# Token blocks folded out of the accumulation bank, early starts for three sequence groups, and magnitudes of half the second weight summed on ScalarE

## The chip, the cores and the metric

The kernel runs on one core of one Trainium2 chip. The metric is the device time of one execution in microseconds (us). The engines are TensorE (PE in the profile, its weight loads PEld), VectorE (DVE), ScalarE (ACT), GpSimd (POOL) and SyncE (SP, which here only issues DMAs).

## The reference, cut to what matters

Three stages run one after the other on batch 2, sequence 768, 8 heads of 64 features (512 features in all). First a decayed linear attention in blocks, then a mixing stage with a Fourier transform over tokens and features and a two-layer network, then a second two-layer network.

```
for b in range(nb):                                     # attention, blocks with a carried state
    intra = (q_b @ k_b^T) * Dmask ; intra = intra @ v_b
    inter = (q_b * lam_pow) @ kv_state
    out_b = intra + inter
    kv_state = lam_block * kv_state + (k_b * rev_pow)^T @ v_b

X = np.fft.fft(x, axis=1) ; X = np.fft.fft(X, axis=2)   # mixing over tokens, then features
u = x + np.real(X)
un = (u - mean(u)) / sqrt(var(u) + 1e-6)
x = u + np.maximum(un @ w1, 0) @ w2                     # first network, w1 512x2048, w2 2048x512

xn = (x - mean(x)) / sqrt(var(x) + 1e-6) * g
out = x + np.maximum(xn @ w3, 0) @ w4                   # second network
```

## The kernel before, in words

Each engine has its own program, written out by hand in the order in which it runs; engines meet through counting semaphores (`wait_ge`). Nothing reorders the work, so an instruction that waits holds back all that stands behind it on its engine.

**Attention.** The tokens go in 6 blocks of 128 (`c`) for 2 batches (`b`), 12 units `u = 2c + b`. For a unit, TensorE makes the scores (L377), VectorE masks them (`masks`, L921), TensorE updates the state (L390) and computes the output rows (L407, L412) into a bank `xps[b]`, counted by `pv_done`. ScalarE copies the bank to `xlow` (blocks 0 to 2) or `xhigh` (blocks 3 to 5) in `x_rows` (L684, counted by `x_done`) and sends the rows to a DRAM copy `x_dram` (L687); then `expand` (L697) writes the new state. Output rows of unit u may be written only when `x_rows` of unit u-2 has freed the bank.

**Fold.** The Fourier transform over tokens uses the symmetry of the sine and cosine: block `c` of the upper half is added to and subtracted from block `c-3` of the lower half by VectorE (`fold_tokens`, L953 and L954, counted by `sf_done`), and then its features are folded by GpSimd (`fold_features`, L1350 and L1351, counted by `fold_done[b]`) or, for the last block of batch 0, by VectorE (L982 and L983, `fold_last`). VectorE's program runs, for each u: `decay_state(u-1)`, `masks(u)`, `grow_state(u-1)`, `fold_tokens(u-1)`, and `largest(0, u-4)` (L965), the largest magnitude in one of the 8 chunks of the first weight.

**Sequence and feature transforms.** `sequence` runs 16 groups f (8 for each batch), each of 3 matmuls of 385 or 384 columns (L475; one for each of three token blocks), into `f1_bank[f % 3]`. ScalarE copies each group out (`y_columns`, L750 to L752, `y_done`). `features(j)` (L494) and `middle_row` (L516) transform over features; ScalarE copies one half (`q_rows`, L765), VectorE combines (`combine`, L1071 to L1077, `fix_row` L1088), GpSimd adds the other rows (`add_rows`, L1437, `addA`) onto rows that it gathered from `x_dram` (L1422). SyncE loads further rows from `x_dram` (L331 on), after a wait for all of `x_out`.

**Normalising.** VectorE's `statistics` (L1106) for the first 512 tokens waits for `addA` of two tiles, `deviation` (L758) is ScalarE's square root, `normalise` is L1138. TensorE transposes the result in `turn(0, k)` (L544), ScalarE copies it out (`turned`, L775) and makes its half-precision part (`x_hi`, L792); VectorE makes the rest (`x_lo`, L1147) and two sums (`x_sum`).

**Weights.** Weights are scaled by a power of two taken from their largest magnitude. `largest` over 8 chunks, `largest_of_all` (L989), then TensorE turns the column of maxima into a row (`spread_rows`, L523), VectorE takes its maximum (`tops`, L995), TensorE spreads it back (`spread_back`, L528), VectorE copies it (`walls`, L1003) and makes the scale (`power_of_two`, L1010 to L1021, `wsc_ready`). Then `up_hi` (ScalarE, L722 and L723) and `up_lo` (VectorE, L1031 and L1032) split a chunk of the first weight in two halves, from sums that GpSimd makes (`up_sums`, L1380 to L1385); `down_hi` (L739) and `down_lo` (L1039) do so for the second weight.

**The networks.** From `pair(0)` on TensorE runs 32 pairs: 7 products each by a seven-multiplication scheme (L555) and, one pair behind, the second layer (`down`, L575). The chunks of the first weight from 3 on are made inside pairs 1 to 6.

## Time and profile before

| what | value |
|---|---|
| median of 3 runs | 613.15 us (612.04 to 613.87) |
| profiled execution, its own time | 613.28 us |
| its span | 611.5 us |
| PE busy | 593.2 us, 97% of the span |
| DVE busy | 369.4 us, 60% |
| ACT busy | 242.5 us, 40% |
| POOL busy | 146.7 us, 24% |
| mean granted TensorE clock | 0.994 |

The page of the profile names, for each engine, how long it was busy in the span, and in 40 slices of the span how busy it was and which share of full clock TensorE was granted. The answers of the trace go finer: the timeline lists instructions in order of time, merged where they repeat, with the idle time before them and what ended it; the table of stretches gives busy time and granted clock of chosen stretches. A line number is that of the kernel before.

### The profile page before, as it was taken

What the parts mean: (1) busy time and instruction counts of PE and PEld (TensorE: products, weight loads), DVE (VectorE), ACT (ScalarE), POOL (GpSimd) and SP (SyncE); (2) the same over time, 40 slices, a digit from 0 to 9 for tenths busy, and PEclk for the clock granted to TensorE, in tenths of its full rate; (3) what the DMA queues carried; (4) which work ended last, traced back from release to release, by engine and by line L of the source; (5) the groups of instructions that cost most, each with busy time, mean ns of one, the idle gap of its engine ahead of it and who ended that gap; (6) DMA issues with size and microseconds to landing.
All of it is one profiled execution on the core that took longest, in us unless ns stands there. A gap on an engine that the chain in (4) does not pass through costs nothing.

```text
span 611.5 us, 10866 instructions
## 1 busy us (share of the span) xinstructions
PE 593.2 (97%) x4143; PEld 404.3 (66%) x4143; DVE 369.4 (60%) x641; ACT 242.5 (40%) x488; POOL 146.7 (24%) x129
## 2 busy tenths in 40 slices
PE   9998899999999999999989999999999999999997
PEld 4898655776565667666656665666666766666664
DVE  2589779987766765665867897624454333433223
ACT  0232153744555223442456664344332344223221
POOL 1646685154231000103034751002000020000000
PEclk9999799999999999999999999999999999999999
DMA  7999880000000643213022422000010000010001
GB/s 234 395 385 388 292 264 0 2 1 1 2 1 1 178 127 111 86 53 105 18 86 70 135 74 70 0 3 0 1 66 5 1 2 1 22 47 1 1 2 69
DMA packets 41412, 50.43 MB, mean 82 GB/s; under 512 B 2442, under 2 KB 28690, under 8 KB 39956
## 3 DMA queue, kind: packets, MB, share of 16 engines
q1 hardware_dynamic: 39156, 45.05, 22.2%
q10 hardware_dynamic: 1728, 3.15, 1.3%
q0 software_dynamic: 480, 1.57, 0.8%
q8 instruction: 32, 0.52, 0.3%
q14 instruction: 16, 0.13, 0.1%
HBM read 43.46 MB, written 6.30 MB: 81 GB/s over the span
## 4 chain that ended last, share of the span: by engine, by line
PE 71%; DVE 10%; POOL 7%; DMA 5%; ACT 3%; issue 3%; SPq 1%; DVEq 0%; POOLq 0%; ACTq 0%
PE bank L575 33%; PE bank L555 30%; DMA arena<-attn 3%; PE bank L412 2%; DVE arena L1031 2%; PE bank L544 2%; DMA arena<-w 1%; PE bank L407 1%; POOL arena L1381 1%; POOL arena L1380 1%; DVE arena L1172 1%; POOL arena L1422 1%; POOL arena L1383 1%; DVE arena L1032 1%; DVE arena L1039 1%
## 5 line engine op out<-in xcount | busy, mean ns | idle before, releaser
L575 PE MATMUL bank<-arena 128*128 128x512 f16 x1152 | 287.1, 379 | 2.8 <-DVE arena L1180 1.5
L555 PE MATMUL bank<-arena 128*128 128x256 f16 x2016 | 259.4, 273 | 2.4 <-DVE arena L1032 1.8
L555 PEld LDWEIGHTS bank<-arena 128*128 128x128 f16 x2016 | 196.6, 98 | 76.7 <-DVE arena L1032 3.3
L575 PEld LDWEIGHTS bank<-arena 128*128 128x128 f16 x1152 | 112.1, 98 | 89.5 <-DVE arena L1180 1.8
L1172 DVE SCALAR_TENSOR_TENSOR arena<-arena 128x512 f16<-128x512 f32 x96 | 72.2, 752 | 67.6 <-ACT arena L808 67.6
L808 ACT ACTIVATE arena<-arena 128x512 f16<-128x512 f32 x96 | 60.4, 629 | 98.5 <-DVE arena L1213 93.1
L1207 DVE SCALAR_TENSOR_TENSOR arena<-bank,arena 128x256 f32<-128x256 f32 x48 | 20.3, 423 | 77.8 <-PE bank L555 77.8
L854 ACT ACTIVATE arena<-bank 128x256 f32<-128x256 f32 x48 | 18.4, 384 | 63.9 <-PE bank L555 63.9
L1393 POOL TENSOR_TENSOR arena<-arena 128x512 f32<-128x512 f32 x5 | 6.8, 1368 | 146.9 <-ACT arena L779 90.8
L1213 DVE SCALAR_TENSOR_TENSOR arena<-bank,arena 128x256 f32<-128x256 f32 x48 | 20.2, 422 | 30.6 <-PE bank L555 30.6
L965 DVE TENSOR_REDUCE arena<-arena 128x1 f32<-128x1024 f32 x32 | 38.4, 1208 | 0.0
L1147 DVE TENSOR_TENSOR arena<-arena 128x512 f16<-128x512 f32 x42 | 30.1, 728 | 10.4 <-ACT arena L792 10.4
L825 ACT ACTIVATE arena<-bank 128x256 f32<-128x256 f32 x48 | 18.4, 384 | 42.1 <-PE bank L555 42.1
L475 PE MATMUL bank<-arena 128*128 128x385 f32 (+1 forms) x96 | 34.5, 512 | 0.0
L1380 POOL TENSOR_TENSOR arena<-arena 128x256 f32<-128x256 f32 x16 | 14.8, 926 | 66.9 <-DMA arena<-w 64.5
L837 ACT ACTIVATE arena<-bank 128x256 f32<-128x256 f32 x48 | 18.4, 382 | 31.3 <-PE bank L555 31.3
L1196 DVE SCALAR_TENSOR_TENSOR arena<-bank,arena 128x256 f32<-128x256 f32 x48 | 20.1, 418 | 17.4 <-PE bank L555 17.3
L820 ACT ACTIVATE arena<-bank 128x256 f32<-128x256 f32 x48 | 18.2, 379 | 28.0 <-PE bank L555 28.0
L412 PE MATMUL bank<-arena 128*128 128x64 f32 x192 | 27.3, 272 | 0.2 <-DVE arena L921 0.2
L475 PEld LDWEIGHTS bank<-arena 128*128 128x128 f32 x96 | 18.6, 200 | 12.4 <-issue 2.2
L412 PEld LDWEIGHTS bank<-arena 128*128 128x128 f32 x192 | 25.9, 199 | 0.7 <-issue 0.7
L792 ACT ACTIVATE arena<-arena 128x512 f16<-128x512 f32 x42 | 25.7, 624 | 0.0
(101 smaller groups left out, 553.4 us busy)
## 6 DMA issues: line engine op xcount, KB each, us to landing
arena<-w SPq DMA_DIRECT2D x48, 256.0 KB, 4.4
arena<-w SPq DMA_DIRECT2D x24, 512.0 KB, 3.7
arena<-attn SPq DMA_DIRECT2D x10, 1024.0 KB, 8.7
x_dram<-arena ACTq DMA_DIRECT2D x12, 256.0 KB, 6.9
out<-arena SPq DMA_DIRECT2D x12, 256.0 KB, 2.1
arena<-attn SPq DMA_DIRECT2D x4, 512.0 KB, 4.3
arena<-c SPq DMA_DIRECT2D x1, 1153.5 KB, 11.1
arena<-g SPq DMA_DIRECT2D x1, 514.0 KB, 12.7
```

What stands on the lines that cost most here:

```text
L412: last = nc.tensor.matmul(xps[b][:, h * D:(h + 1) * D], PT[b][:, par, pair, :], v, start=first, stop=True, skip_group_check=not first)
L475: last = nc.tensor.matmul(f1_bank[f % 3][:, 0:n], lhs, C1[:, c, par * NE:par * NE + n], start=c == 0, stop=c == HALF - 1)
L555: last = nc.tensor.matmul(bank_, wst[:, i, wx, w, kt, :], xs[s % 2][:, ux, x, kt, :], start=not started and k == 0, stop=k == 5, skip_grou ...
L575: last = nc.tensor.matmul(ops[t][:], hT[n % 2][:, half, hx, t * P:(t + 1) * P], wdn[:, i, wx, half * DM:(half + 1) * DM], start=first and ...
L792: nc.scalar.activation(xs[s % 2][:, 0, which, :, :], x_block(which), ACT.Copy).then_inc(xh_done, 1)
L808: nc.scalar.activation(hT[n % 2][:, half, 0, :], z[n % 2][:, half, :], ACT.Relu).then_inc(hh_done, 1)
L965: nc.vector.tensor_reduce(wmax_chunks[:, m, c:c + 1], raw, AX.X, ALU.max, apply_absolute_value=True).then_inc(wred[m], 1)
L1147: nc.vector.tensor_tensor(xs[s % 2][:, 1, which, :, :], x_block(which), xs[s % 2][:, 0, which, :, :], ALU.subtract).then_inc(xl_done, 1)
L1172: nc.vector.scalar_tensor_tensor(hT[n % 2][:, half, 1, :], z[n % 2][:, half, :], 0.0, hT[n % 2][:, half, 0, :], ALU.max, ALU.subtract).the ...
L1207: nc.vector.scalar_tensor_tensor(z[n % 2][:, 1, 0:HT], seventh[:, 0:HT], H_SCALE, u2, ALU.mult, ALU.add).then_inc(z21_out, 1)
L1213: nc.vector.scalar_tensor_tensor(z[n % 2][:, 1, HT:TOK], a, H_SCALE, p7, ALU.mult, ALU.add).then_inc(z22_out, 1)
L1380: nc.gpsimd.tensor_tensor(s1, a21, a22, ALU.add).then_inc(ws_step, 1)
```

## The change

It does the following.

1. `fold_tokens` reads the upper block straight out of the bank `xps[b]` and waits for `pv_done` rather than `x_done`. `x_rows` of units 6 to 11 in turn waits for `sf_done`, so that the copy frees the bank only after the fold, and `expand` comes ahead of it there.
2. `largest(0, 4..7)` moves from the loop's iterations u = 8 to 11 to behind the loop.
3. The first three sequence groups are written as `first_sequence`: their matmuls over token blocks 0 and 1 come first, those over block 2, which wait for `fold_last`, after them. Matmuls are the same in number and shape.
4. `spread_rows(0, 1)` stands behind group 3 (before: 1), `spread_back(0, 1)` behind group 5 (before: 3). Those of the second weight, `(1, 2)`, move from among groups 9 to 11 to behind group 13 and behind `features(2)`, and to bank 7. `turn(0)` stands behind group 12 (before: 13).
5. `magnitude(4..7)` on ScalarE takes the sums of magnitudes (`Abs` with an accumulated output) of four chunks of the second weight; `largest(1, 4..7)` is gone from VectorE. The sum bounds the largest magnitude from above, so the scale may come out smaller.
6. `up_hi(0, 2)` moves behind `y_columns(11)`, `up_lo(0, 1)` behind `normalise`, `up_lo(0, 2)` to the end of pair 0, `down_hi(0, 0)` into pair 0. `largest_of_all(1)`, `tops(1, 2)`, `walls(1, 2)` and `power_of_two(1)` move to behind `normalise` and among and behind `x_lo`.

```diff
+            def along(f, c):
+                b, par, dk = f // 8, f // 4 % 2, f % 4
+                n = NE if par == 0 else NO
+                lhs = fold[:, b, 2 * par + dk // 2, c, (dk % 2) * P:(dk % 2 + 1) * P]
+                return nc.tensor.matmul(f1_bank[f % 3][:, 0:n], lhs, C1[:, c, par * NE:par * NE + n],
+                                        start=c == 0, stop=c == HALF - 1)
+            def first_sequence():
+                pe.wait_ge(fold_done[0], HALF - 1)
+                for f in range(3):
+                    for c in range(HALF - 1):
+                        along(f, c)
+                for f in range(3):
+                    pe.wait_ge(fold_last, 1 + f // 2)
+                    along(f, HALF - 1).then_inc(f1_done, 1)
             def sequence(groups):
                 for f in groups:
-                    b, par, dk = f // 8, f // 4 % 2, f % 4
-                    if f == 0:
-                        pe.wait_ge(fold_done[b], HALF - 1)
-                        pe.wait_ge(fold_last, 1)
-                    if f == 2:
-                        pe.wait_ge(fold_last, 2)
+                    b = f // 8
                     if f == 8:
                         pe.wait_ge(fold_done[b], HALF)
                     if f >= 3:
                         pe.wait_ge(y_done, f - 2)
-                    n = NE if par == 0 else NO
                     for c in range(HALF):
-                        lhs = fold[:, b, 2 * par + dk // 2, c, (dk % 2) * P:(dk % 2 + 1) * P]
-                        last = nc.tensor.matmul(f1_bank[f % 3][:, 0:n], lhs, C1[:, c, par * NE:par * NE + n],
-                                                start=c == 0, stop=c == HALF - 1)
+                        last = along(f, c)
                     last.then_inc(f1_done, 1)
...
-            sequence(range(2))
+            first_sequence()
+            sequence(range(3, 4))
             pe.wait_ge(id_in, 16)
             pe.wait_ge(ones_done, 1)
             spread_rows(0, 1)
-            sequence(range(2, 4))
+            sequence(range(4, 6))
             spread_back(0, 1)
-            sequence(range(4, F1_FIRST))
...
             features(0)
             middle_row(0)
             features(1)
-            sequence(range(F1_FIRST, F1_FIRST + 1))
+            sequence(range(F1_FIRST, F1_FIRST + 4))
             pe.wait_ge(fix_done, 1)
-            spread_rows(1, 2)
-            sequence(range(F1_FIRST + 1, F1_FIRST + 3))
-            spread_back(1, 2)
-            sequence(range(F1_FIRST + 3, 14))
-            pe.wait_ge(wall_done, 2)
             for k in range(KT):
                 turn(0, k)
-            sequence(range(14, 16))
+            sequence(range(F1_FIRST + 4, F1_FIRST + 5))
             pe.wait_ge(ev_done, NT)
+            spread_rows(1, 2, bank[7])
+            sequence(range(F1_FIRST + 5, 16))
             features(2)
+            spread_back(1, 2, bank[7])
...
                 c, b = divmod(u, B)
                 act.wait_ge(pv_done, u + 1)
+                if c >= HALF:
+                    act.wait_ge(sf_done, u - B * HALF + 1)
                 rows_u = xlow[:, b, c, :] if c < HALF else xhigh[:, c - HALF, b, :]
                 nc.scalar.activation(rows_u, xps[b][:], ACT.Copy).then_inc(x_done, 1)
...
                     act.wait_ge(zeroed, B)
+                act.wait_ge(pv_done, u + 1)
                 act.wait_ge(st_done, u + 1)
...
             for u in range(UNITS):
-                x_rows(u)
-                if u < UNITS - B:
+                if u < B * HALF:
+                    x_rows(u)
                     expand(u)
+                else:
+                    if u < UNITS - B:
+                        expand(u)
+                    x_rows(u)
...
                     if c == 2:
-                        act.wait_ge(fold_done[0], HALF - 1)
-                        act.wait_ge(fold_done[1], HALF)
+                        act.wait_ge(mag_done, SLOTS // 2)
...
+            def magnitude(c):
+                act.wait_ge(w_chunk_in[1][c], 16)
+                if c > SLOTS // 2:
+                    act.wait_ge(mag_done, c - SLOTS // 2)
+                junk = wst[:, 2, 0, 0:4, :, :].rearrange("p b k n -> p (b k n)")
+                nc.scalar.activation(junk, wraw[1][:, c, :], ACT.Abs,
+                                     accum_out=wmax_chunks[:, 1, c:c + 1]).then_inc(mag_done, 1)
...
                 hidden_hi(n, 1)
+                if n == 0:
+                    down_hi(0, 0)
...
             y_columns(7)
+            act.wait_ge(fold_done[0], HALF - 1)
+            act.wait_ge(fold_done[1], HALF)
+            magnitude(4)
             y_columns(8)
+            magnitude(5)
             q_rows(0)
+            magnitude(6)
+            q_rows(1)
+            y_columns(9)
+            magnitude(7)
+            deviation(0)
+            y_columns(10)
+            y_columns(11)
             up_hi(0, 2)
-            q_rows(1)
-            for f in range(9, 12):
-                y_columns(f)
-            deviation(0)
             y_columns(12)
-            y_columns(13)
             for k in range(KT):
                 turned(0, k)
             x_hi(0, 0)
             x_hi(0, 1)
+            x_hi(0, 2)
+            y_columns(13)
+            x_hi(0, 3)
+            x_hi(0, 4)
             y_columns(14)
-            x_hi(0, 2)
-            x_hi(0, 3)
+            x_hi(0, 5)
+            x_hi(0, 6)
             y_columns(15)
-            x_hi(0, 4)
-            x_hi(0, 5)
-            down_hi(0, 0)
-            x_hi(0, 6)
             q_rows(2)
...
             def fold_tokens(u):
                 c, b = divmod(u, B)
-                dve.wait_ge(x_done, u + 1)
+                dve.wait_ge(pv_done, u + 1)
                 if c > HALF + 1:
                     dve.wait_ge(fold_done[b], c - HALF - 1)
                 to = sfold[c % 2]
-                lo, hi = xlow[:, b, c - HALF, :], xhigh[:, c - HALF, b, :]
+                lo, hi = xlow[:, b, c - HALF, :], xps[b][:]
                 nc.vector.tensor_tensor(to[:, b, 0, :], lo, hi, ALU.add)
                 nc.vector.tensor_tensor(to[:, b, 1, :], lo, hi, ALU.subtract).then_inc(sf_done, 1)
...
-                if UNITS - SLOTS <= u < UNITS:
-                    largest(0, u - UNITS + SLOTS)
+                if 2 * B <= u < 2 * B + SLOTS // 2:
+                    largest(0, u - 2 * B)
+            for c in range(SLOTS // 2, SLOTS):
+                largest(0, c)
             def largest_of_all(m):
-                dve.wait_ge(wred[m], SLOTS)
+                if m == 1:
+                    dve.wait_ge(mag_done, SLOTS // 2)
+                dve.wait_ge(wred[m], SLOTS // 2 if m == 1 else SLOTS)
...
                 hidden_lo(n, 0)
+                if n == 0:
+                    up_lo(0, 2)
...
-            for c in range(2, 5):
-                largest(1, c)
+            largest(1, 2)
+            largest(1, 3)
             up_lo(0, 0)
-            largest(1, 5)
-            up_lo(0, 1)
-            largest(1, 6)
-            largest(1, 7)
-            largest_of_all(1)
             combine(0)
             fix_row(0)
             combine(1)
-            tops(1, 2)
             statistics(0, range(NT))
-            walls(1, 2)
             row_scale(0)
             normalise(0, range(NT))
-            up_lo(0, 2)
+            largest_of_all(1)
+            up_lo(0, 1)
             x_sum(0, 0)
             x_sum(0, 1)
             x_lo(0, 0)
             x_lo(0, 1)
             x_sum(0, 2)
-            power_of_two(1)
             x_lo(0, 2)
             x_sum(0, 3)
+            tops(1, 2, bank[7])
             for k in range(3, 7):
                 x_lo(0, k)
+            walls(1, 2, bank[7])
+            power_of_two(1)
             out_scale(0)
```

VectorE's program at the end of the attention loop, before (L921 `masks`, L953 and L954 `fold_tokens`, L965 `largest`, L982 and L983 the last feature fold):

```order
L953 TENSOR_TENSOR arena<-arena 128x512 [waits x_done]
L954 TENSOR_TENSOR arena<-arena 128x512
L965 TENSOR_REDUCE arena<-arena 128x1 [waits w0_in6]
L921 TENSOR_TENSOR arena<-bank,arena 128x512 [waits pv_done,qk_done]
L921 TENSOR_TENSOR arena<-bank,arena 128x512
L953 TENSOR_TENSOR arena<-arena 128x512 [waits fold_done0,x_done]
L954 TENSOR_TENSOR arena<-arena 128x512
L982 TENSOR_TENSOR arena<-arena 128x2x256 [waits sf_done]
L983 TENSOR_TENSOR arena<-arena 128x2x256
L965 TENSOR_REDUCE arena<-arena 128x1 [waits w0_in7]
L953 TENSOR_TENSOR arena<-arena 128x512 [waits fold_done1,x_done]
L954 TENSOR_TENSOR arena<-arena 128x512
```

and with the change (L951 `masks`, L983 and L984 `fold_tokens`, L1012 and L1013 the last feature fold, L995 `largest`; L1023 is `largest_of_all`):

```order
L983 TENSOR_TENSOR arena<-arena,bank 128x512 [waits pv_done]
L984 TENSOR_TENSOR arena<-arena,bank 128x512
L951 TENSOR_TENSOR arena<-bank,arena 128x512 [waits pv_done,qk_done]
L951 TENSOR_TENSOR arena<-bank,arena 128x512
L983 TENSOR_TENSOR arena<-arena,bank 128x512 [waits fold_done0,pv_done]
L984 TENSOR_TENSOR arena<-arena,bank 128x512
L1012 TENSOR_TENSOR arena<-arena 128x2x256 [waits sf_done]
L1013 TENSOR_TENSOR arena<-arena 128x2x256
L983 TENSOR_TENSOR arena<-arena,bank 128x512 [waits fold_done1,pv_done]
L984 TENSOR_TENSOR arena<-arena,bank 128x512
L995 TENSOR_REDUCE arena<-arena 128x1 [waits w0_in4]
L995 TENSOR_REDUCE arena<-arena 128x1 [waits w0_in5]
```

Two more L995 rows and then L1023 follow. The masks of unit 11 follow the fold of unit 9 with no reduction between, the fold reads the bank, and four reductions stand behind the last fold.

TensorE's program from the second `features` to `turn(0)` and on to the last group, before (L475 sequence, L523 `spread_rows`, L528 `spread_back`, L544 `turn`):

```order
L475 MATMUL bank<-arena 128x385 x2
L523 MATMUL bank<-arena 1x128 [waits wmax_done,fix_done]
L475 MATMUL bank<-arena 128x385 [waits y_done]
L475 MATMUL bank<-arena 128x385 x2
L475 MATMUL bank<-arena 128x385 [waits y_done]
L475 MATMUL bank<-arena 128x385 x2
L528 MATMUL bank<-arena 128x1 [waits top_done]
L475 MATMUL bank<-arena 128x384 [waits y_done]
L475 MATMUL bank<-arena 128x384 x2
L475 MATMUL bank<-arena 128x384 [waits y_done]
L475 MATMUL bank<-arena 128x384 x2
L544 MATMUL bank<-arena 128x128 [waits un_done,wall_done]
```

and with the change (L461 sequence, L552 `turn`, L531 `spread_rows`):

```order
L461 MATMUL bank<-arena 128x384 [waits y_done]
L461 MATMUL bank<-arena 128x384 x2
L552 MATMUL bank<-arena 128x128 [waits un_done,fix_done]
L552 MATMUL bank<-arena 128x128 x15
L461 MATMUL bank<-arena 128x384 [waits y_done]
L461 MATMUL bank<-arena 128x384 x2
L531 MATMUL bank<-arena 1x128 [waits wmax_done,ev_done]
L461 MATMUL bank<-arena 128x384 [waits y_done]
L461 MATMUL bank<-arena 128x384 x2
L461 MATMUL bank<-arena 128x384 [waits y_done]
L461 MATMUL bank<-arena 128x384 x2
```

Four groups (9 to 12) now stand between the second `features` and `turn(0)`, before five with two small matmuls; three groups and one small matmul stand behind it, before two groups.

## Rows read from the trace of the kernel before

**Rows 1.** The page: span, and the granted clock in 40 slices.

```profile
span 611.5 us, 10866 instructions
...
PEclk9999799999999999999999999999999999999999
```

**Rows 2.** Timeline of PE, end of attention: start us, us, engine line op, idle before.

```profile
58.35 1.16 PE L377 MATMUL bank<-arena 64*128 64x128 f32 x16
60.59 0.46 PE L407 MATMUL bank<-arena 128*128 128x128 f32 x2 [1.08 <-DVE arena L921]
...
66.30 0.46 PE L407 MATMUL bank<-arena 128*128 128x128 f32 x2 [2.84 <-DVE arena L921]
```

**Rows 3.** Table of stretches: us; PE, PEld, DVE, ACT, POOL busy; PEclk; DMA share; GB/s.

```profile
64.00:66.00 2.00, 0.00 (x0) 0.00 (x0) 2.00 (x3) 0.09 (x1) 2.00 (x2) 1.00 1.05 399
68.00:70.00 2.00, 2.00 (x11) 2.00 (x11) 1.97 (x4) 0.00 (x0) 0.00 (x0) 0.50 0.37 142
```

**Rows 4.** Timeline of DVE, the last iterations of its loop.

```profile
60.70 1.45 DVE L953 TENSOR_TENSOR arena<-arena 128x512 f32<-128x512 f32 x1
62.08 1.75 DVE L954 TENSOR_TENSOR arena<-arena 128x512 f32<-128x512 f32 x1
63.75 1.21 DVE L965 TENSOR_REDUCE arena<-arena 128x1 f32<-128x1024 f32 x1
64.88 1.27 DVE L921 TENSOR_TENSOR arena<-bank,arena 128x512 f32<-128x512 f32 x2
...
68.46 0.69 DVE L982 TENSOR_TENSOR arena<-arena 128x512 f32<-128x512 f32 x1
```

**Rows 5.** Timeline of PE, from the first sequence group to pair 0.

```profile
70.46 5.96 PE L475 MATMUL bank<-arena 128*128 128x385 f32 x12
...
76.66 4.15 PE L475 MATMUL bank<-arena 128*128 128x385 f32 x12
...
90.83 1.95 PE L494 MATMUL bank<-arena 128*128 128x129 f32 x16
...
95.56 2.11 PE L475 MATMUL bank<-arena 128*128 128x385 f32 x6
...
106.93 1.94 PE L544 MATMUL bank<-arena 128*128 128x128 f32 x16 [0.19 <-DVE arena L1138]
...
114.37 4.33 PE L555 MATMUL bank<-arena 128*128 128x256 f16 x36
```

**Rows 6.** Timeline of DVE and ACT, scale of the first weight and its first chunk.

```profile
81.15 0.16 DVE L1003 COPY arena<-bank 128x1 f32<-128x1 f32 x1 [2.67 <-PE bank L528]
...
83.86 1.15 ACT L722 ACTIVATE arena<-arena 128x1024 f16<-128x1024 f32 x1
...
85.74 0.36 ACT L751 ACTIVATE arena<-bank 128x256 f32<-128x256 f32 x1
86.01 0.26 ACT L752 ACTIVATE arena<-bank 128x128 f32<-128x128 f32 x1
```

**Rows 7.** Timeline of DVE, first combine, second combine, statistics.

```profile
94.89 0.42 DVE L1071 TENSOR_TENSOR arena<-bank,arena 128x257 f32<-128x257 f32 x1
...
97.79 0.41 DVE L1071 TENSOR_TENSOR arena<-bank,arena 128x257 f32<-128x257 f32 x1
...
100.50 2.47 DVE L1106 BATCH_NORM_STATS2 arena<-arena 128x6 f32<-128x512 f32 x4 [0.20 <-POOL arena L1437]
```

**Rows 8.** Timeline of POOL and SP, last fold and reading back from DRAM.

```profile
72.70 1.27 POOL L1350 TENSOR_TENSOR arena<-arena 128x512 f32<-128x512 f32 x1 [4.83 <-DVE arena L954]
...
81.25 1.12 POOL L1422 DMA_INDIRECT arena<-x_dram,arena  x1 [0.34 <-issue]
...
76.44 0.25 SPq L331 DMA_DIRECT2D arena<-x_dram  x1
```

**Rows 9.** Timeline of DVE in pair 1 and of PE in pair 5, idle time.

```profile
127.93 0.42 DVE L1213 SCALAR_TENSOR_TENSOR arena<-bank,arena 128x256 f32<-128x256 f32 x1 [0.88 <-PE bank L555]
...
167.78 2.14 PE L555 MATMUL bank<-arena 128*128 128x256 f16 x18 [0.80 <-DVE arena L1032]
```

19 lines of the change are left out of this document (10 added, 9 removed).

## The prediction

> **What bounds the kernel now.** I read the page first, then the timeline of TensorE with its idle times, then the timelines of the engines that end those idle times. By the page TensorE is busy in 97% of the span and its granted clock is full in all slices but one, the fifth [rows 1]. So a change helps only by what it takes out of TensorE's own line: idle time, time at the lower clock, or work. The timeline shows where the line is broken in the stretch that the change touches: 1.08 us before the output rows of unit 10 and 2.84 us before those of unit 11, both ended by L921, VectorE's masks [rows 2]. Behind the second gap the granted clock falls from 1.00 to 0.50, that is from 2.4 to 1.2 GHz [rows 3]. The lower clock shows in durations: the rows of unit 10 took 66.30 - 2.84 - 60.59 = 2.87 us, those of unit 11 took 70.46 - 66.30 = 4.16 us [rows 2, 5], so 1.3 us more; and the first two sequence groups took 76.66 - 70.46 = 6.2 us, the next two 4.15 us [rows 5], so 2.05 us more (with a small matmul in them). From there to pair 0 TensorE has only small gaps, 0.2 us of them before the transpose [rows 5]. Inside the pairs some gaps are left, 0.80 us the longest, set by VectorE's own work in the pair [rows 9]; they keep their place relative to pair 0 and should move with it.
>
> Why VectorE is late there: the masks of unit 11 (64.88) stand behind the fold of unit 9, 1.45 + 1.75 us, and a reduction of 1.21 us [rows 4].
>
> **The change, part by part.**
>
> *Fold out of the bank, reductions moved.* No row shows a fold with one operand in the bank. The nearest is L921, which has a bank operand, the same 512 columns, and ran while GpSimd was busy all the time: 1.27 us for two [rows 3, 4]. The other end is the fold as it stands, 3.2 us for the two. L982 shows what two SBUF operands cost once GpSimd is idle, 0.69 us [rows 3, 4]. I take 1.3 us. The Trainium skill, "SBUF — State Buffer", section "Who interferes with whom", says that a VectorE instruction with two SBUF inputs contends with GpSimd, and one with at most one does not; the rows agree, 1.75 against 0.69 us with and without GpSimd and 0.64 us beside it with a bank operand. By that rule the sum is 608.8 us; were it not so, the sum would be that of the third rival.
>
> Step by step: unit 9's rows end at 58.35; its fold ends at 59.7, the masks of unit 11 at 61.0. TensorE has the scores of unit 11 (1.1 us) and the rows of unit 10 (2.87 us) until 62.3, so it waits for neither. Both gaps go, and with them, I take it, the lower clock. Attention ends at 58.35 + 1.1 + 2 x 2.87 = 65.2 instead of 70.46: 5.3 us. The added wait of `x_rows` for the fold holds bank and ScalarE only until 60.4, before unit 11 needs the bank; what is queued behind it on ScalarE, the DRAM write, is 1.3 us later relative to TensorE.
>
> *Early start of three groups.* Without the early part TensorE would need `fold_last` at 65.2. The fold of unit 10 runs 62.3 to 63.6 and the two of L982's kind end between 65.0 (0.69 us each) and 67.1 (1.75 us each). The twelve instructions over blocks 0 and 1 last 4 us, to 69.2, and cover either. No stall, and the amount of work is the same. With the full clock the next 2.05 us are saved: TensorE is 7.4 us ahead, 0.4 us more with the small gaps.
>
> *Where that lead is given back.* First, the scale of the first weight. VectorE now does four reductions behind the last fold: fold 67.1 to 68.4, then 4 x 1.13 us (63.75 to 64.88 is one [rows 4]), maxima ready at 73.1. TensorE has done four groups (8.1 us) at 73.3, so the price is 0 to 0.2 us; I put in 0.2. It sends the maximum back after two more groups, at 77.8; the copy and the chain of small instructions of 0.16 us each [rows 6] make some 1.2 us: scale at 79.0. ScalarE then has `up_hi` 1.88 us, a group's copy 0.53 us [rows 6], a second copy, `up_hi` again and a third copy, in all 5.4 us, until 84.4. `features(0)` needs that third copy, and TensorE arrives at 65.2 + (90.83 - 70.46 - 2.05) + 0.2 = 83.7. Stall 0.7 to 1 us; start 84.6, before 90.83.
>
> Second, the way to the transpose. The two features and the middle row take 95.56 - 90.83 = 4.73 us [rows 5], so end at 89.3, `features(0)` alone at 86.5. ScalarE stands behind two magnitudes. No row shows one; the nearest are L722, 1024 columns in 1.15 us [rows 6], and VectorE's reduction, 1.21 us [rows 4]; below nothing it cannot cost, above I allow double. I take 1.15 us. Then the first combine starts at about 87.6. From the first combine to the second it took 97.79 - 94.89 = 2.9 us, then 2.71 us to the statistics, and 6.43 us from there to the transpose [rows 5, 7]. Of these, none had to wait for TensorE. So: second combine 90.6, statistics 93.3, transpose 99.7 to 99.8. Before, VectorE took 2.2 us from the end of the features to the second combine, with chunk reductions ahead of it; now 1.3 us. TensorE arrives after four groups, at 89.3 + 8.2 = 97.5. New stall: 2.3 us.
>
> Third, from transpose to pair 0: 114.37 - 106.93 = 7.44 us before [rows 5]; now a third group, 2.0 us, and two small matmuls with what surrounds them, 0.6 us. Pair 0 starts at 109.85 instead of 114.37.
>
> *The way through DRAM* has to keep up. The last fold ends at 68.4 and frees GpSimd's last fold; from that (72.70) to the first gather (81.25) it took 8.55 us [rows 8], so 77.0, and gathers, sums and `add_rows(0)` are done by 91. The write of the last rows landed 76.44 - 70.46 = 6.0 us after TensorE's last row [rows 5, 8]; from 68.4 that is 74.4. Neither is late. On SyncE's queue the loads of the second weight's last four chunks start with the last row and are 5 us earlier too.
>
> *Into pairs 0 and 1.* `up_lo(0, 2)` goes to VectorE's end of pair 0, `down_hi(0, 0)` to ScalarE's pair 0. VectorE has idle time there, 0.88 us of it before one instruction [rows 9], and `up_lo(0, 2)` is needed only by pair 2. Price between 0 and its length, about 2.3 us; I take 0, being nearest to a row with idle time on VectorE and none on TensorE. `down_hi` delays a copy by 1.15 us; cover is the first product of pair 1 and a feature step on TensorE, 1.5 us. If that cover is gone, it costs up to 1.15 us. The magnitudes and the moved small matmuls cost TensorE nothing elsewhere.
>
> **Sum.** 613.28 (the profiled execution's own time, 0.13 us above the median of 613.15) - 7.4 - 0.4 + 0.2 + 0.8 + 2.3 = 608.8 us; the reading by pair 0, 114.37 - 109.85 = 4.5 us, gives the same.
>
> **The rivals.**
>
> *The clock falls again.* For it: the new stall of 2.3 us before the transpose is not far from the 2.84 us that preceded the fall [rows 2, 3]. Against it: 0.80 us in the pairs and 1.08 us alone did nothing. Price: 1.3 + 2.05 = 3.35 us, as before. 612.1 us. The Trainium skill, "TensorE: Matmul & The Clock Gate", section "Part 4: PE-mode transpose", says that transposes do not count as activity in the same way; the work right behind this stall is 1.9 us of transposes, which by that rule lengthens the lull to some 4.2 us. In the trace of before they follow 0.19 us of idle time and the clock stays up, which tells nothing on it. Chance 0.17.
>
> *VectorE and ScalarE keep pace.* If the way from features to transpose shortens with the reductions gone and ScalarE's chain is quicker, the 2.3 us stall falls to nothing: 606.5 us. Against it: the 9.1 us from combine to transpose are a chain of instructions each waiting for the last. Chance 0.12.
>
> *The fold stays slow.* With 3.2 us for a fold, unit 11's masks end at 62.8 and the maxima 2.5 us later; the scale and all behind it come some 2 us later. 610.9 us. Chance 0.05.
>
> *The transpose does not come earlier.* It now has one group more and 0.6 us of small pieces behind it, so pair 0 starts 10.05 us after it, not 7.44. If the rows through DRAM, `add_rows` on GpSimd, or `deviation` on ScalarE hold it at 106.9, the kernel is 2.6 us slower: 615.9 us. It decides from a transpose later than 106.2 for over 0.3% slower. For it: gathers and last write are one chain behind the new wait of `x_rows`, and ScalarE's order puts magnitudes ahead of the copies that this chain needs. Against it: by the rows that chain has 2 us to spare. Chance 0.06.
>
> **How the numbers follow.** 0.3%, 1.8 us, is about what a measurement can tell from no change. My forecast, 608.8 us, has 0.60; with the second and third rival, faster has 0.77; the fallen clock, within 1.8 us of before, gives 0.17 for same; slower 0.06. The range goes from 606.2 (no stall before the transpose) to 612.4 (the fallen clock).
>
> **What would show it.** Right: no idle before the last two units' rows, clock 1.00 from 64 to 76, attention over at about 65, folds of 0.65 us each, a stall of about 2 us before the transpose ended by L1172 (`normalise`), pair 0 at about 110. Wrong: a granted clock of 0.50 anywhere, a stall of over a microsecond before the third copy or at `spread_rows`, or pairs that are longer than before.

## The result, and the profile after

The change takes the median from 613.87 us to 609.95 us (7 runs of each; 613.15 us was the median of the first three before); the ratio is 0.9925, with a 95% interval of 0.9903 to 0.9946. One of the 7 took 616.87 us, which the ratio leaves out as slow; with an eighth run, of 609.04 us, in its place the median is 609.04 us. Two repeats beside fresh runs of the kernel before gave 609.29 us (ratio 0.9943, 0.9917 to 0.9970) and 609.12 us (0.9939, 0.9920 to 0.9958). It is faster by 0.6 to 0.75%, about 4 us. The forecast was 608.8 us with a range of 606.2 to 612.4.

The first profiled execution of the changed kernel was disturbed in the attention loop by a load that came late, and took 616.87 us. Single runs as long came again, not traced: one of 12 in the first repeat, 616.43 us at a mean clock of 0.986, and one of 29 of the kernel before beside it, 619.46 us at 0.983. GpSimd waited for keys and values, TensorE waited for GpSimd, and the granted clock went to 0.50. One of those waits on the timeline (start, us, engine line op, idle before) and a stretch of 5 us behind it in the table of stretches (eighth column: granted clock):

```profile
23.68 0.69 PE L390 MATMUL bank<-arena 128*64 128x64 f32 x16 [2.53 <-POOL arena L1371]
```

```profile
25.00:30.00 5.00, 5.00 (x27) 4.88 (x27) 2.27 (x1) 0.32 (x1) 2.56 (x2) 0.50 1.06 372
```

The readings below are therefore from the profile of the first repeat, whose own time is 609.60 us (span 607.8), and of the second, 608.36 us (span 606.6). The page of the first repeat, to set beside [rows 1]:

```profile
span 607.8 us, 10888 instructions
...
PE 591.7 (97%) x4143; PEld 403.6 (66%) x4143; DVE 366.6 (60%) x637; ACT 246.1 (40%) x496; POOL 141.1 (23%) x129
...
PEclk9999998999999999999999999999999999999999
```

The lower clock of the fifth slice is gone, and a weaker one stands in the seventh. TensorE's timeline in the first repeat (start, us, engine line op, idle before; L461 is the sequence, L502 and L516 features, L552 the transpose, L563 a product), to set beside [rows 2, 5, 9]:

```profile
64.10 7.98 PE L461 MATMUL bank<-arena 128*128 128x385 f32 x24
...
83.18 2.02 PE L502 MATMUL bank<-arena 128*128 128x129 f32 x16 [0.40 <-ACT arena L765]
...
97.97 2.56 PE L552 MATMUL bank<-arena 128*128 128x128 f32 x16 [2.06 <-DVE arena L1172]
100.33 3.20 PE L461 MATMUL bank<-arena 128*128 128x384 f32 x6
...
109.93 4.10 PE L563 MATMUL bank<-arena 128*128 128x256 f16 x36
114.56 1.48 PE L563 MATMUL bank<-arena 128*128 128x256 f16 x12 [0.52 <-DVE arena L1247]
...
118.89 1.16 PE L516 MATMUL bank<-arena 128*128 128x129 f32 x8 [0.65 <-ACT arena L787]
...
163.88 2.14 PE L563 MATMUL bank<-arena 128*128 128x256 f16 x18 [0.80 <-DVE arena L1066]
```

Attention ends at 64.10 instead of 70.46, with no idle time before the last two units' rows. `features(0)` waits 0.40 us for ScalarE, the transpose 2.06 us for VectorE's `normalise`, pair 0 starts at 109.93 instead of 114.37, and in pair 1 there is a new gap of 0.65 us, ended by L787, ScalarE's copy of `q_rows`. The 0.80 us gap in pair 5 is the old one [rows 9].

The transposes took 2.56 us and the group behind them 3.20 us for 1.94 and 2.10 us of work. The table of stretches says why:

```profile
98.00:100.00 2.00, 2.00 (x15) 2.00 (x16) 2.00 (x3) 1.52 (x4) 0.00 (x0) 0.78 0.00 0
100.00:102.00 2.00, 2.00 (x6) 1.33 (x5) 1.42 (x3) 1.75 (x4) 1.84 (x3) 0.50 0.00 0
```

In the second repeat the same gap did not bring the clock down, and the way from transpose to pair 0 took 10.28 us where it took 11.96 us above, 1.68 us less:

```profile
64.77 7.98 PE L461 MATMUL bank<-arena 128*128 128x385 f32 x24
...
98.65 1.94 PE L552 MATMUL bank<-arena 128*128 128x128 f32 x16 [2.06 <-DVE arena L1172]
100.43 2.10 PE L461 MATMUL bank<-arena 128*128 128x384 f32 x6
...
108.93 4.10 PE L563 MATMUL bank<-arena 128*128 128x256 f16 x36
```

VectorE at the end of its loop (L983 and L984 are the fold, L1012 and L1013 the last feature fold), to set beside [rows 4]:

```profile
57.71 0.69 DVE L983 TENSOR_TENSOR arena<-arena,bank 128x512 f32<-128x512 f32 x1 [0.96 <-PE bank L412]
58.31 0.68 DVE L984 TENSOR_TENSOR arena<-arena,bank 128x512 f32<-128x512 f32 x1
...
62.94 1.35 DVE L1012 TENSOR_TENSOR arena<-arena 128x512 f32<-128x512 f32 x1
64.22 1.75 DVE L1013 TENSOR_TENSOR arena<-arena 128x512 f32<-128x512 f32 x1
```

The two instructions of a fold take 0.69 and 0.68 us beside a busy GpSimd, where they took 1.45 and 1.75 us, while the last feature fold, with two operands in SBUF, still takes 1.35 and 1.75 us.

### The profile page after: what moved, and what is told of

It is laid out like the page before. It is cut to its first block, busy times and chain, and to the rows that moved or that the text cites. A ratio compares the mean times of both kernels' runs of the same rounds, so it can differ in the third digit from the quotient of the medians.

```text
span 615.1 us, 10888 instructions
## 1 busy us (share of the span) xinstructions
PE 597.8 (97%) x4143; PEld 410.1 (67%) x4143; DVE 361.1 (59%) x637; ACT 245.9 (40%) x496; POOL 141.2 (23%) x129
## 4 chain that ended last, share of the span: by engine, by line
PE 76%; DVE 10%; ACT 4%; DMA 3%; issue 3%; POOL 2%; SPq 1%; DVEq 0%; ACTq 0%; POOLq 0%
PE bank L583 33%; PE bank L563 30%; PE bank L412 3%; PE bank L461 3%; PE bank L407 2%; DVE arena L1065 2%; DMA arena<-attn 2%; PE bank L377 2%; PE bank L552 2%; DVE arena L1206 1%; DVE arena L1066 1%; DVE arena L1073 1%; PE bank L390 1%; ACT arena L830 1%; DVE arena L1181 1%
## 5 line engine op out<-in xcount | busy, mean ns | idle before, releaser
L563 PE MATMUL bank<-arena 128*128 128x256 f16 x2016 | 259.2, 273 | 2.4 <-DVE arena L1066 1.8
L563 PEld LDWEIGHTS bank<-arena 128*128 128x128 f16 x2016 | 196.7, 98 | 76.3 <-DVE arena L1066 3.3
L1181 DVE TENSOR_TENSOR arena<-arena 128x512 f16<-128x512 f32 x42 | 31.7, 764 | 10.4 <-ACT arena L814 10.4
L995 DVE TENSOR_REDUCE arena<-arena 128x1 f32<-128x1024 f32 x28 | 33.5, 1208 | 0.0
L461 PE MATMUL bank<-arena 128*128 128x385 f32 (+1 forms) x96 | 32.4, 490 | 0.0
L1412 POOL TENSOR_TENSOR arena<-arena 128x256 f32<-128x256 f32 x16 | 13.2, 824 | 76.7 <-DMA arena<-w 65.5
L412 PE MATMUL bank<-arena 128*128 128x64 f32 x192 | 29.3, 286 | 0.0
L412 PEld LDWEIGHTS bank<-arena 128*128 128x128 f32 x192 | 28.5, 216 | 0.2
L461 PEld LDWEIGHTS bank<-arena 128*128 128x128 f32 x96 | 17.7, 189 | 11.7 <-issue 0.6
```

The lines of the kernel that those rows point to most:

```text
L412: last = nc.tensor.matmul(xps[b][:, h * D:(h + 1) * D], PT[b][:, par, pair, :], v, start=first, stop=True, skip_group_check=not first)
L461: return nc.tensor.matmul(f1_bank[f % 3][:, 0:n], lhs, C1[:, c, par * NE:par * NE + n], start=c == 0, stop=c == HALF - 1)
L563: last = nc.tensor.matmul(bank_, wst[:, i, wx, w, kt, :], xs[s % 2][:, ux, x, kt, :], start=not started and k == 0, stop=k == 5, skip_grou ...
L995: nc.vector.tensor_reduce(wmax_chunks[:, m, c:c + 1], raw, AX.X, ALU.max, apply_absolute_value=True).then_inc(wred[m], 1)
L1181: nc.vector.tensor_tensor(xs[s % 2][:, 1, which, :, :], x_block(which), xs[s % 2][:, 0, which, :, :], ALU.subtract).then_inc(xl_done, 1)
```

## The experiments

Times are medians; a ratio is to the kernel before on the same chip, with its 95% interval. As the attention loop wanders by up to a microsecond from one execution to the next (waits of GpSimd for loads), places further on are best compared as distances from the end of attention, which is the start of the first sequence group. "The fall" is the granted clock going from 1.00 to 0.50. One fall behind the transposes gives a mean clock of 0.997 (the profile of the first repeat); mean clocks are given for runs without a trace too, but they do not say where in the run the clock fell.

### The change again

> The changed kernel once more, to have a profile in which the attention loop is not disturbed. My account (the lead of 7.8 us by TensorE's gaps and lower clock, of which 3.3 us is given back before pair 0, plus 0.65 us in pair 1 seen in the first profile): TensorE ends attention at about 65.2 us, clock 1.00 throughout, stall before the transpose 2 us, pair 0 at about 109.5, time 607.5 to 608.5 where the clock is 1.000. Rival (the first profile is typical, and the attention loop now has a gap at 21 us behind which the clock falls): the fall is there again, attention ends after 70, time over 612.

Measured: 609.29 us; attention over at 64.10, no fall there; pair 0 at 109.93. Of 12 runs 4 had a mean clock of 1.000 and took 607.75 to 608.11 us; 6 with 0.997 to 0.999 took 609.09 to 609.6 us; the last two took 611.6 us at 0.994 and 616.43 us at 0.986. The rival, that the disturbed profile is typical, falls: a run as long as the disturbed one came once in 12. What the expectation missed is the fall behind the transposes, which the profile shows and which the clock of 0.997 in 5 of the 12 runs fits.

### The fold and the reductions of the loop alone

```diff
 # in the kernel before, parts 1 and 2: fold_tokens from xps[b], x_rows behind sf_done, expand first, and
-                if UNITS - SLOTS <= u < UNITS:
-                    largest(0, u - UNITS + SLOTS)
+                if 2 * B <= u < 2 * B + SLOTS // 2:
+                    largest(0, u - 2 * B)
+            for c in range(SLOTS // 2, SLOTS):
+                largest(0, c)
```

> The kernel before with only parts 1 and 2 of the change (fold out of the bank, x_rows after the fold, four reductions of the first weight behind the loop). Theory A (the whole lead comes from the two gaps and the clock): attention ends at 65.2, clock 1.00, but the first sequence groups wait for fold_last, up to 2 us, and the maxima stand at 73, three groups' worth of TensorE work after its spread_rows place behind group 1 (69.3 or later), so TensorE stalls there 2 to 4 us; the transpose is reached 3 to 5 us earlier than before; time 609 to 611. Theory B (the moves further on carry the gain): no more than 1 us of gain, 612.5 or more.

Measured: 612.17 us, ratio 0.9980 (0.9952 to 1.0008): no gain that can be told. TensorE's timeline (L475 sequence, L523 `spread_rows`) and the stretch behind it:

```profile
65.76 4.12 PE L475 MATMUL bank<-arena 128*128 128x385 f32 x12 [0.66 <-DVE arena L989]
73.33 0.58 PE L523 MATMUL bank<-arena 128*1 128x128 f32 x2 [3.46 <-DVE arena L998]
...
107.27 1.94 PE L544 MATMUL bank<-arena 128*128 128x128 f32 x16 [0.20 <-DVE arena L1147]
```

```profile
70.00:72.00 2.00, 0.00 (x0) 0.00 (x0) 2.00 (x3) 0.70 (x5) 2.00 (x3) 1.00 1.06 392
74.00:76.00 2.00, 2.00 (x4) 1.08 (x5) 1.82 (x4) 0.00 (x0) 1.96 (x3) 0.50 0.59 222
```

Attention is over at 65.1 (65.76 less the wait of 0.66), as theory A says, and the stall of 3.46 us at `spread_rows` is in its range too. But behind that stall the clock falls, just as it did behind the old gap. The transpose starts at 107.27, 0.3 us later than before [rows 5]. The gap was moved, not removed. So by themselves parts 1 and 2 bring nothing that can be told, and theory A missed twice: the transpose did not come 3 to 5 us earlier, and the median lies above its 609 to 611, as it left the fall out. What parts 3, 4 and 6 bring one by one was not tried, apart from the place of the transpose below.

### The slow fold in the changed kernel

```diff
-                dve.wait_ge(pv_done, u + 1)
+                dve.wait_ge(x_done, u + 1)
-                lo, hi = xlow[:, b, c - HALF, :], xps[b][:]
+                lo, hi = xlow[:, b, c - HALF, :], xhigh[:, c - HALF, b, :]
 # and x_rows, expand in their old order, without the wait for sf_done
```

> The changed kernel with the fold as before (waits for x_done and reads xhigh; x_rows and expand in their old order). Theory A (the bank operand frees VectorE from waiting for GpSimd): each fold takes up to 3.2 us again, masks of unit 11 some 2 us later, attention ends at 66 to 67 with a gap of 0.5 to 1.5 us, the maxima about 2.5 us later, time 610 to 611. Theory B (only the reductions that were taken out of the loop mattered): within 0.5 us of the changed kernel.

Measured: 614.54 us, ratio 1.0031 (1.0011 to 1.0051), 5.3 us above the changed kernel on the same chip, and slower than the kernel before.

```profile
60.10 0.46 PE L407 MATMUL bank<-arena 128*128 128x128 f32 x2 [1.00 <-DVE arena L944]
...
64.67 0.46 PE L407 MATMUL bank<-arena 128*128 128x128 f32 x2 [1.71 <-DVE arena L944]
...
67.37 7.98 PE L461 MATMUL bank<-arena 128*128 128x385 f32 x24
...
101.26 3.29 PE L552 MATMUL bank<-arena 128*128 128x128 f32 x16 [2.07 <-DVE arena L1165]
```

Both gaps are back, 1.00 and 1.71 us, and attention ends at 67.37, 3.3 us later than with the bank operand. The reductions taken out of the loop do not do it alone: theory B falls. Theory A has the mechanism and is short on size, by 3.5 us: it left out the gap before unit 10. The profiled run, 612.82 us, is one of the fastest: it is 3.2 us longer than the profile of the first repeat, which is what attention lost, and both have one fall, behind the wait of 2.06 or 2.07 us (transposes 3.29 us here). In 9 of the 12 runs the mean clock was 0.994 or less, lower than one such fall gives, and none had 1.000; where the clock fell in those runs no trace shows. The experiment undoes three things together, the operand, the wait for the copy and the order on ScalarE, and does not tell them apart.

### One group more before the transpose

```diff
-            sequence(range(F1_FIRST, F1_FIRST + 4))
+            sequence(range(F1_FIRST, F1_FIRST + 5))
```

> The changed kernel with turn(0) behind group 13, as before, in place of behind group 12. Theory A (the transpose is held at 99.8 by combine, statistics and normalise, and TensorE idles 2.1 us there): group 13 fills the idle time, the stall falls to 0.3 us or less, the transpose starts at the same time and pair 0 about 2.0 us earlier; ratio to the changed kernel 0.9967. Rival (group 13 waits for ScalarE's copy of group 10, which stands behind the square root, so that group 13 starts late and pushes the transpose): transpose up to 2 us later, no gain in total.

Measured: 607.07 us, ratio 0.9912 (0.9882 to 0.9942), 2.2 us below the changed kernel on the same chip; clock 1.000 in 5 of 6 runs.

```profile
64.27 7.98 PE L461 MATMUL bank<-arena 128*128 128x385 f32 x24
...
98.16 1.94 PE L552 MATMUL bank<-arena 128*128 128x128 f32 x16
...
107.15 0.38 PE L536 MATMUL bank<-arena 1*128 1x1 f32 x2 [0.89 <-DVE arena L1031]
107.83 4.10 PE L563 MATMUL bank<-arena 128*128 128x256 f16 x36 [0.30 <-ACT arena L765]
```

The transpose starts 33.89 us behind the end of attention, and in both repeats of the change 33.87 and 33.88: it is held by the chain, and group 13 costs nothing ahead of it. But 1.19 us of the 2.06 come back, 0.89 at `spread_back` (L536, waiting for VectorE's `tops`) and 0.30 before pair 0. Pair 0 lies 43.56 us behind the end of attention instead of 44.16. The rest of the 2.2 us, more than half, is by the clocks the fall that does not come; the intervals of the two ratios (0.9882 to 0.9942 and 0.9917 to 0.9970) overlap.

### One group less before the transpose

```diff
-            sequence(range(F1_FIRST, F1_FIRST + 4))
+            sequence(range(F1_FIRST, F1_FIRST + 3))
```

> The changed kernel with turn(0) behind group 11 in place of 12, so that the idle time before the transpose is doubled to about 4.1 us. Theory A (the transpose is chain-bound, and a gap of this size brings the clock down in every run): the transpose starts at the same time, 98.0, one group more stands behind it (2.05 us), and the clock falls in all or nearly all runs at a price of 1.7 to 3.4 us; time 611.5 to 613.5, no run at clock 1.000. Rival (the falls seen behind the transposes in part of the runs have nothing to do with the gap): 2.05 us more than the changed kernel, and the same mix of clocks as there, a third of the runs at 1.000.

Measured: 613.48 us, ratio 1.0018 (0.9997 to 1.0038); none of 12 runs at 1.000, 7 at 0.997.

```profile
66.41 7.98 PE L461 MATMUL bank<-arena 128*128 128x385 f32 x24
...
100.28 3.41 PE L552 MATMUL bank<-arena 128*128 128x128 f32 x16 [4.00 <-DVE arena L1172]
```

The wait is 4.00 us, the transposes take 3.41 us, and again they start 33.87 us behind the end of attention. Theory A holds: with 4.00 us no run kept the clock at 1.000, with 2.06 us about half did. Of the time, 0.67 us is a new wait at `spread_rows`, ended by ScalarE's copy of the transposed tiles.

### The old gap filled

```diff
             rows(last_block, 0, 1, False)
+            pe.wait_ge(st_done, UNITS - B)
+            for _ in range(3):
+                nc.tensor.matmul(bank[7][:], blk_in[1][:, 0, 0, :], blk_in[1][:, 0, 0:4, :]..., start=True, stop=True)
             rows(last_block, 1, 1, False)
```

> The kernel before with three added 512-column matmuls (results thrown away, into bank 7) in the 2.84 us gap before unit 11's rows. Nothing else moves, so the rows still start at 66.3. Theory A (the gap brings the clock down, and the fall costs 3.35 us apart from the gap itself): granted clock 1.00 there, rows of unit 11 in 2.9 us, time 609.5 to 610.5, ratio 0.9945. Rival (the clock falls for another reason, or what it gives back is caught by a later wait): within 1 us of before.

Measured: 609.68 us against 612.38 us of the kernel before on that chip, ratio 0.9971 (0.9946 to 0.9996). It does the work of before and three matmuls more.

```profile
65.75 0.46 PE L407 MATMUL bank<-arena 128*128 128x128 f32 x2 [0.22 <-DVE arena L925]
...
68.75 4.12 PE L479 MATMUL bank<-arena 128*128 128x385 f32 x12
...
73.11 4.15 PE L479 MATMUL bank<-arena 128*128 128x385 f32 x12
...
102.72 1.91 PE L548 MATMUL bank<-arena 128*128 128x128 f32 x16
```

The rows of unit 11 take 3.0 us, the first two groups 4.36 us with the small matmul: no fall, as theory A says, and the small waits of before by the transpose are gone. The kernel before had itself run on this chip at a clock of 0.997 in 8 of 31 runs, which may be why the gain of the medians, 2.7 us, is less than 3.35 us; three of the 12 filled runs took 612.79 to 615.12 us. A fall thus has a price of its own, here 1.8 us by the ratio and 2.7 us by the medians, where the whole change brings about 4 us. By its interval the ratio could also be a gain of 0.2 or of 3.3 us.

### The reductions back on VectorE

```diff
             up_lo(0, 0)
+            for c in range(SLOTS // 2, SLOTS):
+                largest(1, c)
 # and no magnitude(4..7) on ScalarE
```

> The changed kernel with part 5 undone: chunks 4 to 7 of the second weight are reduced on VectorE again, behind up_lo(0, 0), and ScalarE makes no magnitudes. Theory A (magnitudes on ScalarE free VectorE for the first combine, as the change has it): VectorE is free at 82.3 and has 3.6 us until the first combine, four reductions take 4.6 us, so combine starts up to 1.0 us later, transpose up to 1 us later; time 0.5 to 1 us longer than the changed kernel. Rival (ScalarE's magnitudes hold the copy that combine waits for, 1.3 us of them between features(0) and the copy): the two even out, within 0.4 us of the changed kernel.

Measured: 610.84 us, ratio 0.9979 (0.9960 to 0.9998), on another chip than the changed kernel's 0.9943 and 0.9939.

```profile
65.03 7.98 PE L461 MATMUL bank<-arena 128*128 128x385 f32 x24
...
99.79 2.44 PE L552 MATMUL bank<-arena 128*128 128x128 f32 x16 [2.91 <-DVE arena L1166]
```

The transpose starts 34.76 us behind the end of attention, 0.88 us later than with the magnitudes, and waits 2.91 us: theory A's range for the transpose; the rival, that it evens out, falls. No run of 12 had a clock of 1.000. By the ratios the time is about 0.4% longer, 2.2 us or more, above theory A's 0.5 to 1 us: the longer gap costs more than its length.

### The copy that a feature step waits for

```diff
                 nc.scalar.activation(p7, seventh[:, 0:HT], ACT.Copy, scale=H_SCALE).then_inc(p7_out, 1)
+                if n == 1:
+                    down_hi(0, 1)
...
-                if s == 0 and i < SLOTS - 1:
+                if s == 0 and 0 < i < SLOTS - 1:
```

> The changed kernel with ScalarE's down_hi(0, 1) behind the copy of the seventh product in pair 1, in place of the end of pair 0. Theory (the 0.65 us gap in pair 1 is down_hi(0, 0) and (0, 1) standing ahead of the copy that a feature step waits for): the gap goes and the time falls by 0.65 us against the changed kernel. Rival (VectorE or another copy ends the wait next): less than 0.2 us.

Measured: 608.76 us, ratio 0.9943 (0.9919 to 0.9967), which runs on another chip can't tell from the change. The trace can:

```profile
117.60 1.48 PE L563 MATMUL bank<-arena 128*128 128x256 f16 x12 [0.52 <-DVE arena L1249]
...
135.10 0.82 PE L583 MATMUL bank<-arena 128*128 128x512 f16 x3 [0.24 <-DVE arena L1075]
...
166.59 2.14 PE L563 MATMUL bank<-arena 128*128 128x256 f16 x18 [0.80 <-DVE arena L1068]
```

The 0.65 us gap is gone and a new one of 0.24 us stands at 135.10, ended by L1075, VectorE's `down_lo`. From the first gap in pair 0 to that in pair 5 it takes 48.99 us, with the change 49.32 us: half of the 0.65 us stays. This profiled run took 611.8 us at a clock of 0.994, yet its transposes, behind the same wait of 2.06 us, took 1.94 us. Its clock was 0.50 much earlier, in attention from 26 to 32 us. So not every run below 1.000 fell behind the transposes.

### Two combinations

The first joins group 13 ahead of the transpose, the later `down_hi(0, 1)`, and `up_lo(0, 1)` in VectorE's idle time before the first combine.

```diff
             up_lo(0, 0)
+            up_lo(0, 1)
             combine(0)
...
             largest_of_all(1)
-            up_lo(0, 1)
```

> The changed kernel with turn(0) behind group 13, up_lo(0, 1) in VectorE's idle time before the first combine (82.3 to 85.9 there), and down_hi(0, 1) inside pair 1. Expected if the waits at spread_back (0.9 us) and before pair 0 (0.3 us) come from VectorE's chain of sums and x_lo behind up_lo(0, 1) and beside GpSimd's sums: VectorE's chain ends 1.5 to 2 us earlier, these waits fall to 0.3 us or less, the 0.65 us gap in pair 1 goes, clock 1.000 in most runs; time 605 to 606. Rival (up_lo(0, 1) there pushes the first combine, or the chain hangs on the transpose alone): 606.5 or more.

The second adds the copy of group 15 ahead of the last two `x_hi`, and `spread_back(1, 2)` inside pair 0:

```diff
-            spread_back(1, 2, bank[7])
...
                 product(n, chain[1 - n % 2], A12, B21, False, p2_done)
+                if n == 0:
+                    spread_back(1, 2, bank[7])
```

> As the kernel before this one, and with ScalarE's copy of group 15 ahead of its last two x_hi, and TensorE's spread_back(1, 2) inside pair 0 behind the second product. If what is left of the waits before pair 0 is these two, another 0.3 to 0.5 us is gained over the other. Rival (pair 0 then waits inside for x_lo or for the copies): no difference, and idle time inside pair 0.

Measured: 607.31 us, ratio 0.9913 (0.9885 to 0.9941), and 606.35 us, ratio 0.9888 (0.9864 to 0.9912), on the same chip.

```profile
63.85 7.98 PE L461 MATMUL bank<-arena 128*128 128x385 f32 x24
...
98.26 1.94 PE L552 MATMUL bank<-arena 128*128 128x128 f32 x16 [0.35 <-DVE arena L1174]
...
106.60 4.10 PE L563 MATMUL bank<-arena 128*128 128x256 f16 x36
111.23 1.48 PE L563 MATMUL bank<-arena 128*128 128x256 f16 x12 [0.52 <-DVE arena L1249]
```

```profile
64.64 7.98 PE L461 MATMUL bank<-arena 128*128 128x385 f32 x24
...
112.02 1.48 PE L563 MATMUL bank<-arena 128*128 128x256 f16 x12 [0.52 <-DVE arena L1250]
```

The waits at `spread_back` and before pair 0 are gone. The transpose is 0.5 us later (34.41 us behind the end of attention), since `up_lo(0, 1)` does push the first combine, as the rival has it; yet pair 0 starts 42.75 us behind the end of attention instead of 44.16. Still, 607.31 us is not the 605 to 606 that was expected, and within the rival's 606.5 or more; two of the six runs had a clock of 0.991 and 0.997. For the second, the last product of pair 0 (L563 behind 0.52 us) starts 47.38 us behind the end of attention in both: its rival holds, nothing is gained there. All its runs had a clock of 0.999 or 1.000, four of the other's six, which fits the medians. The second has the lowest median of the kernels here; its interval overlaps with those of the first and of group 13 alone.

### The new gap filled

```diff
             pe.wait_ge(fix_done, 1)
+            pe.wait_ge(de_done, 2)
+            for _ in range(3):
+                nc.tensor.matmul(bank[7][:, 0:NE], C1[:, 0, 0:P], C1[:, 0, 0:NE], start=True, stop=True)
             for k in range(KT):
                 turn(0, k)
```

> The changed kernel with three added 385-column matmuls (results thrown away, into bank 7) in the 2.06 us gap before the transpose. Theory A (the falls of the clock that two runs in three of the changed kernel show come from this gap): the transpose starts at the same time, the clock is 0.999 to 1.000 in nearly all runs, and the median goes to the fastest third of the changed kernel's runs, 1.5 us below its median. Rival (the clock falls for other reasons, such as a late load in the attention loop): the mix of clocks and the median stay as they are.

> The changed kernel beside the one before this on the same chip. By my account its median lies 1 to 2 us above that of the filled kernel, with two thirds of its runs below clock 1.000; by the rival the two have the same median.

Measured on one chip: filled 608.15 us, the change 609.12 us. All six filled runs had a clock of 0.999 or 1.000; of the change's six, three had, with 607.78 to 608.6 us, and three had 0.996 or 0.997, with 609.65 to 609.71 us. The filled transposes start at 98.29, where those of the change beside it start at 98.65. The median is 0.97 us lower, just short of the 1 to 2 us expected, and the intervals of the two ratios overlap (0.9910 to 0.9946 and 0.9920 to 0.9958), so the evidence is the clocks more than the medians. Taken together, 12 of the changed kernel's 26 runs had a clock of 0.999 or 1.000, with a median of 608.1 us, and 10 had 0.996 or 0.997, with 609.6 us: a fall costs 1.5 us or so. The other 4 were lower; of these one was traced, the first profile, and it fell in attention. Of the 24 runs of the four kernels that leave 0.35 us or less of this gap (this one, group 13 ahead, the two combinations), 21 had 0.999 or 1.000.

## Why the prediction was right

Sign and size were right: 608.8 us forecast, 609.1 to 610.0 us measured. The path was right too, but part of the closeness is luck. The forecast has the clock full throughout; the runs in which it stayed full took 608.1 us, 0.7 us less than forecast, and those with one fall 609.6 us. The forecast lies between the two: terms set somewhat too long and a fall left out partly cancel. Two of the prediction's own signs of being wrong were met: a granted clock of 0.50 in some runs, and pairs longer than before. By its own steps:

1. **Attention.** Forecast to end at 65.2; it ended at 64.10 and 64.77. (The lead is added up as 7.4 us; its terms, 5.26 and 2.05 us, give 7.3.) Both gaps and the fall went. The fold was priced at 1.3 us from the masks' row; it takes 1.37 us.
2. **Early groups.** No wait for `fold_last`, with the twelve instructions as cover. Without them the wait was 0.66 us (parts 1 and 2 alone). The later `spread_rows` matters more: at the old place TensorE waited 3.46 us and lost the clock again.
3. **What was given back.** Before `features(0)` 0.8 us forecast, 0.40 us measured: ScalarE's third copy ended 18.9 us behind the end of attention, for 19.2 in the forecast. Before `spread_rows` 0.2 us forecast, none. Before the transpose 2.3 us forecast, 2.06 us measured. These terms were sized rightly to 0.4 us each, and the chain behind them was the right one: the transpose starts 33.9 us behind the end of attention whatever TensorE does in between.
4. **Pairs 0 and 1.** Put at 0, with the price named should the cover of `down_hi` be gone. It was partly gone: 0.65 us, a mis-sized term. I had weighed only the copy behind `down_hi(0, 0)`; the wait came one step later. `down_hi(0, 1)` stood ahead of the copy of `q_rows(3)` before as well, but now both `down_hi` lie between pair 0's first gap and that copy, which starts 3.90 us behind the gap (118.46 less 114.56) instead of 3.18 us (122.40 less 119.22). From pair 0's start to the gap in pair 5 it takes 53.95 us instead of 53.41, so the pairs are 0.54 us longer. ScalarE before (L739 `down_hi`, L765 the copy) and in the first repeat (L752, L787):

```profile
121.10 1.13 ACT L739 ACTIVATE arena<-arena 128x1024 f16<-128x1024 f32 x1
...
122.40 0.38 ACT L765 ACTIVATE arena<-bank 128x257 f32<-128x257 f32 x1
```

```profile
115.13 1.13 ACT L752 ACTIVATE arena<-arena 128x1024 f16<-128x1024 f32 x1
...
117.16 1.13 ACT L752 ACTIVATE arena<-arena 128x1024 f16<-128x1024 f32 x1
...
118.46 0.37 ACT L787 ACTIVATE arena<-bank 128x257 f32<-128x257 f32 x1
```

5. **The clock.** This was the rival with a chance of 0.17, and by the clocks it came about in 10 of 26 runs, at most in 13. The step that failed is the price: I gave it 3.35 us, the whole of what it had cost in attention, and it costs 1.5 to 1.7 us. So it moved the median by a microsecond or less rather than taking most of the gain. My argument against it, that 0.80 and 1.08 us gaps did nothing, was of no use for one of 2.06 us. The rule of the Trainium skill, "TensorE: Matmul & The Clock Gate", section "Part 4: PE-mode transpose", that transposes do not count as activity in the same way, is neither shown nor excluded: a gap of this size was never tried with ordinary matmuls behind it. With ordinary matmuls behind them, gaps of 2.84 us (before) and 3.46 us (parts 1 and 2 alone) came with a fall, and one of 1.71 us (slow fold, its profiled run) did not.
6. **The slow fold** was given 610.9 us; measured on its own it is 614.5 us. The bank operand, with the order that goes with it, carries more than I gave it, for without it the gap before unit 10 is back as well. The rule of the Trainium skill, "SBUF — State Buffer", section "Who interferes with whom", holds in the rows shown: 0.69 and 0.68 us with one operand in the bank, up to 1.75 us with both in SBUF, both beside a busy GpSimd. One row of the kernel before does not show the slowing, a fold's first half with both operands in SBUF:

```profile
66.07 0.67 DVE L953 TENSOR_TENSOR arena<-arena 128x512 f32<-128x512 f32 x1
```

It took 0.67 us though GpSimd's records (1.26 us from 64.91, 1.74 us from 66.13) leave it no idle time there.

The rivals that VectorE and ScalarE keep pace and that the transpose comes no earlier did not occur.

## What to carry to other kernels

Gaps on the bounding engine are moved more easily than removed: after each edit, look for the next wait on that engine and price it with what the clock does behind it, over several runs, since one profile shows only one outcome. Where TensorE must wait for a chain that it cannot shorten, put independent work there, one group more before the transpose here; it delayed nothing and lowered the median by 2.2 us, of which 0.6 us is the gap itself. A VectorE operand read from the accumulation bank instead of its copy in SBUF spared the instruction the wait for the copy, and it took 0.69 us where it had taken up to 1.75 us beside GpSimd; which of the two brought more was not told apart.

## What the runs showed that was not expected

A gap of 2.06 us before the transposes brought the granted clock from 1.00 to 0.50 in some executions of one kernel and not in others (transposes 2.56 us and 1.94 us in the two repeats); with one of 2.91 us and one of 4.00 us none of 12 runs each kept a mean clock of 1.000. Work that is thrown away, three matmuls in a gap of 2.84 us, made the kernel before faster, with a ratio of 0.9971 (0.9946 to 0.9996), while the whole change reached 0.9925 to 0.9943.
